# Letting the first sequence's gathers wait for fewer stores, and projecting its values one row block later instead of two

## The reference

```
y  = scale * q (gamma * state + k v^T)       # retention, 8 heads of 64, token by token
e  = argmax(x @ w_gate), or the expert of the token before where sigmoid(x @ w_local) >= 0.5
x1 = p[e] * relu(x @ w1[e]) @ w2[e]          # 8 experts, 512 -> 1024 -> 512, one for each token
for each of 4 attention experts:             # heads of 64
    ye = softmax(causal(q k^T / 8)) v wo     # q, k, v = x1 @ wq, wk, wv
    out += (top-2 gate weight of the token) * ye
```

## Time and profile before

| | |
|---|---|
| median of 3 runs | 447.73 us (447.07 to 449.4) |
| the profiled execution's own time | 449.13 us |
| its span in the trace | 447.6 us |
| mean granted TensorE clock | 0.969 |
| TensorE busy | 408.5 us (91%) |

### The profile page before, as it was taken

How to read it: one execution, slowest core, us unless ns; L and a number is a source line. 1 busy time by engine, 2 the same in 40 slices (tenths; PEclk the granted TensorE clock), 3 DMA queues, 4 the chain that set the end, 5 groups by cost and what they waited for, 6 DMA issues and landing times.

```text
span 447.6 us, 9522 instructions
## 1 busy us (share of the span) xinstructions
PE 408.5 (91%) x3224; PEld 364.9 (82%) x3225; DVE 251.7 (56%) x483; ACT 231.0 (52%) x500; POOL 78.6 (18%) x100
## 2 busy tenths in 40 slices
PE   6999894497999999999999999399899899989987
PEld 5887883396999999898989897299877789978875
DVE  1667778765474646464646465236777531676740
ACT  4766664154464646454545454134566552466643
POOL 1011113011010101000000000550188400025330
PEclk9999998589999999999999999689999999999999
DMA  8958793776867677776766840452200021220003
GB/s 266 346 187 266 260 404 138 256 233 237 281 234 252 240 265 232 252 245 253 237 232 234 287 183 23 140 166 73 70 1 1 1 95 48 70 70 0 0 0 141
DMA packets 32392, 77.47 MB, mean 173 GB/s; under 512 B 3824, under 2 KB 4080, under 8 KB 32368
## 3 DMA queue, kind: packets, MB, share of 16 engines
q1 hardware_dynamic: 25552, 57.94, 38.5%
q0 software_dynamic: 4224, 14.68, 9.6%
q10 hardware_dynamic: 2592, 4.53, 2.7%
HBM read 56.17 MB, written 17.83 MB: 165 GB/s over the span
## 4 chain that ended last, share of the span: by engine, by line
PE 77%; issue 10%; DMA 6%; POOL 2%; DVE 2%; ACT 1%; POOLq 1%; SPq 0%; ACTq 0%; DVEq 0%
PE bank L1233 7%; PE bank L1231 7%; PE bank L1232 7%; PE bank L1218 6%; PE bank L1217 6%; PE bank L1216 6%; PE bank L1335 5%; PE bank L1320 4%; PE bank L1302 3%; PE bank L1306 3%; PE bank L1277 3%; PE bank L1276 2%; PE bank L1278 2%; POOL tokens_by_expert L446 2%; DMA tokens_by_expert<-zero 2%
## 5 line engine op out<-in xcount | busy, mean ns | idle before, releaser
L1216 PE MATMUL bank<-xh,w1h 128*128 128x256 f32 x256 | 73.6, 288 | 0.9 <-DVE xl L897 0.9
L1217 PE MATMUL bank<-xl,w1h 128*128 128x256 f32 x256 | 73.4, 287 | 0.0
L1218 PE MATMUL bank<-xh,w1l 128*128 128x256 f32 x256 | 73.4, 287 | 0.0
L891 DVE TENSOR_TENSOR w2l<-raw,w2h 128x1024 fp32r<-128x1024 f32 x32 | 37.1, 1222 | 42.9 <-ACT w2h L576 42.9
L576 ACT ACTIVATE w2h<-raw 128x1024 fp32r<-128x1024 f32 x32 | 31.8, 1050 | 48.2 <-PE bank L1233 45.7
L1216 PEld LDWEIGHTS bank<-xh,w1h 128*128 128x128 f32 x256 | 50.2, 196 | 1.3 <-DVE xl L897 1.0
L1231 PE MATMUL bank<-w2h,hh 128*128 128x512 f32 x128 | 50.6, 396 | 0.0
L1217 PEld LDWEIGHTS bank<-xl,w1h 128*128 128x128 f32 x256 | 50.2, 196 | 0.3
L1218 PEld LDWEIGHTS bank<-xh,w1l 128*128 128x128 f32 x256 | 50.1, 196 | 0.0
L1233 PE MATMUL bank<-w2h,hl 128*128 128x512 f32 x128 | 49.9, 390 | 0.0
L1232 PE MATMUL bank<-w2l,hh 128*128 128x512 f32 x128 | 49.8, 389 | 0.0
(11 more groups left out here) (159 smaller groups left out, 865.6 us busy)
## 6 DMA issues: line engine op xcount, KB each, us to landing
raw<-in_w SPq DMA_DIRECT2D x64, 512.0 KB, 5.7
tokens_by_expert<-zero POOLq DMA_DIRECT2D x8, 512.0 KB, 6.2
xr<-tokens_by_expert POOLq DMA_DIRECT2D x8, 512.0 KB, 4.0
outputs_by_expert<-ysb ACTq DMA_DIRECT2D x16, 256.0 KB
kt_in<-in_kT SPq DMA_DIRECT2D x12, 256.0 KB
q_in<-in_qT SPq DMA_DIRECT2D x12, 256.0 KB
out<-osb SPq DMA_DIRECT2D x12, 256.0 KB, 2.0
v_in<-in_vR SPq DMA_DIRECT2D x11, 256.0 KB, 4.9
```

Source lines behind the costliest of these rows:

```text
L891: dve.tensor_tensor(part(low), raw[:, q, :], part(high).bitcast(F32), ALU.subtract).then_inc(w_lo, 1)
L1216: pe.matmul(to, w1h[:, dc, at], xh[:, dc, :], start=(dc == 0), stop=False)
L1217: pe.matmul(to, w1h[:, dc, at], xl[:, dc, :], start=False, stop=False)
L1218: last = pe.matmul(to, w1l[:, dc, at], xh[:, dc, :], start=False, stop=(dc == DC - 1))
```

## The change

The stores get one semaphore for each half (`ey_stored[0]`, `ey_stored[1]`), and the zeroing one of its own. While counting, VectorE keeps the counts at the end of the first sequence (`seq_count`). TensorE turns them into a row beside the final counts, VectorE copies the number of first-sequence rows in the last expert, and works out from it and from the last expert's first tile how many stores of each half GpSimd must see before the first sequence's rows are all there (`seq_i`). GpSimd loads both numbers into registers, waits for the two semaphores, and gathers the first sequence; it waits for `all_stored` only before it gathers the second. One more tile of `ys` is zeroed. ScalarE waits for the zeroing once, behind the exponentials of the routing. On TensorE and ScalarE the values of block `t` of the first sequence come after block `t + 1` is turned.

```diff
-CLEARED = MAX_TILES - E
+CLEARED = MAX_TILES - E + 1
...
+    small[:, C_HALVES:C_HALVES + TH * MAXH] = (TILE * np.arange(MAXH)[None, :] + P * np.arange(TH)[:, None]).reshape(-1)
+    small[:, C_HALVES] = -1.0
...
-            for g in range(E, MAX_TILES):
+            for g in range(MAX_TILES - CLEARED, MAX_TILES):
-                sp.dma_start(rows(ys, g * TILE, TILE)..., zero[:, :]).then_inc(ey_stored, 16)
+                sp.dma_start(rows(ys, g * TILE, TILE)..., zero[:, :]).then_inc(ys_cleared, 16)
...
             pool.wait_ge(pos2_ready, 1)
-            pool.wait_ge(all_stored, 1)
+            pool.wait_ge(seq_ready, 1)
+            tiles = [pool.value_load(seq_i[0:1, th:th + 1], min_val=E - th, max_val=MAX_TILES) for th in range(TH)]
+            for th in range(TH):
+                pool.wait_ge(ey_stored[th], 16 * tiles[th] + 16)
+            pool.sem_inc(seq_stored, 1)
+            pool.wait_ge(seq_stored, 1)
...
             gather(0)
+            pool.wait_ge(all_stored, 1)
             gather(1)
...
-                act.wait_ge(ey_stored, 16 * CLEARED + 16 * TH * (n - 1))
                 for th in range(TH):
+                    act.wait_ge(ey_stored[th], 16 * n)
...
-                    act.dma_start(rows(ys, row, P), ysb[:, th, :]).then_inc(ey_stored, 16)
+                    act.dma_start(rows(ys, row, P), ysb[:, th, :]).then_inc(ey_stored[th], 16)
...
             act.activation(exps[:, :, :], exps[:, :, :], ACT.Exp).then_inc(exps_ready, 1)
+            act.wait_ge(ys_cleared, 16 * CLEARED)
+            for th in range(TH):
+                act.sem_inc(ey_stored[th], 16)
...
-            act.wait_ge(ey_stored, 16 * CLEARED + 16 * TH * (tb + nt))
+            for th in range(TH):
+                act.wait_ge(ey_stored[th], 16 * (tb + nt) + 16)
             act.sem_inc(all_stored, 1)
...
-            for t in range(C + 2):
+            for t in range(C + 1):
                 if t < C:
                     split_x2(0, t)
-                if t >= 2:
-                    values(0, t - 2)
+                if t >= 1:
+                    values(0, t - 1)
...
+                if g == closing[C - 1]:
+                    dve.tensor_copy(seq_count[:, :], cnt[:, s, w - 1:w]).then_inc(seq_counted, 1)
...
+            dve.tensor_copy(seq_row[:, 0:1], bank[0:1, 6, 2 * E - 1:2 * E]).then_inc(seq_step, 1)
...
+            dve.wait_ge(seq_step, 1)
+            dve.tensor_tensor(seq_over[:, :], seq_row[:, 0:1].to_broadcast([1, TH * MAXH]),
+                              cst[0:1, C_HALVES:C_HALVES + TH * MAXH], ALU.is_gt).then_inc(seq_step, 1)
+            dve.wait_ge(seq_step, 2)
+            dve.reduce_sum(seq_row[:, 1:1 + TH], seq_over[:, :].rearrange("o (h k) -> o h k", h=TH), AX.X).then_inc(seq_step, 1)
+            dve.wait_ge(seq_step, 3)
+            dve.tensor_tensor(seq_i[:, :], seq_row[:, 1:1 + TH],
+                              route_f[:, R_TB + E - 1:R_TB + E].to_broadcast([1, TH]), ALU.add).then_inc(seq_ready, 1)
...
+            pe.wait_ge(seq_counted, 1)
             pe.wait_ge(cnt_ready, last_g + 1)
+            pe.matmul(bank[0:1, 6, E:2 * E], seq_count[:, :], ident[0:E, 0:E], start=True, stop=True)
...
-            for t in range(C + 2):
+            for t in range(C + 1):
                 if t < C:
                     turn_x2(0, t)
-                if t == 2:
+                if t == 1:
                     pe.wait_ge(m2_lo, 2)
-                if t >= 2:
-                    project_values(0, t - 2)
+                if t >= 1:
+                    project_values(0, t - 1)
```

More of the change, by code:

```diff
@@ L55 @@
 C_PADMIN = C_PICK + 1 + E
-C_N = C_PADMIN + E
+C_HALVES = C_PADMIN + E
+MAXH = S // TILE
+C_N = C_HALVES + TH * MAXH
 L_CAUSAL, L_KD, L_CG = 0, P, P + H
@@ L140, in build_kernel @@
         over = sb("over", [1, E * MAXT])
+        seq_count = sb("seq_count", [E, 1])
+        seq_row = sb("seq_row", [1, 1 + TH])
+        seq_over = sb("seq_over", [1, TH * MAXH])
+        seq_i = sb("seq_i", [1, TH], I32)
         ones = sb("ones", [E, GMAX * P])
@@ L241, in build_kernel @@
         ey_done, ey_ready = sem("ey_done"), sem("ey_ready")
-        ey_stored, all_stored = sem("ey_stored"), sem("all_stored")
+        ys_cleared, all_stored = sem("ys_cleared"), sem("all_stored")
+        ey_stored = [sem(f"ey_stored{th}") for th in range(TH)]
+        seq_counted, seq_step, seq_ready, seq_stored = (
+            sem("seq_counted"), sem("seq_step"), sem("seq_ready"), sem("seq_stored"))
         delta_ready, pos2_step, pos2_ready = (
@@ L397, in _ @@
             sp.wait_ge(zeroed, 1)
-            for g in range(E, MAX_TILES):
-                sp.dma_start(rows(ys, g * TILE, TILE).rearrange("(p a) n -> p (a n)", p=P), zero[:, :]).then_inc(ey_stored, 16)
+            for g in range(MAX_TILES - CLEARED, MAX_TILES):
+                sp.dma_start(rows(ys, g * TILE, TILE).rearrange("(p a) n -> p (a n)", p=P), zero[:, :]).then_inc(ys_cleared, 16)
             for s in range(XRING):
```

## The result

The changed kernel takes 444.78 us in the median of 12 runs (440.89 to 447.68), the kernel before 447.61 in 12 runs (445.3 to 449.4). The ratio is 0.9927, with a 95% interval of 0.9905 to 0.9949: 2.3 to 4.3 us faster. The longest of the 12 runs, 447.68, counts as one in the chip's slower state and isn't in the ratio. Forecast were 442.8 and a gain of 4.9. The time lies within the range of 439.8 to 445.8, but above the 441.8 to 444.5 of the forecast rival A. The gain by the ratio, 3.3 us, is two thirds of the forecast.

What follows compares the result with a forecast made beforehand. TensorE was taken as the bound, busy for 91% of the span with 77% of the chain. The profiled 449.13 - 5.0 + 0.1 gave 444.2; from the median 447.73 the same sum gave 442.8, range 439.8 to 445.8.

Steps and rivals of the forecast that it cites:

- rival A: Hand-over from experts to attention: the clock falls, gain 4 to 5.5 us, about 442.8; chance 0.50.
- The new wait opens 5.4 us earlier: GpSimd's wait before the first sequence's gathers: first gather at 277.33, TensorE's first turn at 281.20, 5.4 us earlier.
- Rival C: GpSimd's new wait opens no earlier; only the shorter lag's 0.4 us is left, 447.3; chance 0.06.
- ScalarE's copy, held by the store: ScalarE's first copy of a turned block waits for the second half's store until 282.6; first values at 284.0.
- the store gets only what the gathers leave: Late bound for the second half's store beside the gathers: its DMA part takes 2.0 us, landing at 283.2.
- half rate: Second half's store beside the gathers, with queues taking turns: slowed to about half rate at most, landing at 282.5.
- The clock: TensorE's clock at the hand-over: somewhat likelier than not to fall, then 4.3 us at half clock lose 2.15.
- Part 2: First sequence's values one block late instead of two: worth about 0.4 to 0.6 us, contained in the 284.0.
- The additions: Small added work, as zeroing, counting and register set-up, lies beside other work: +0.1 us, bounds 0 and 0.8.
- D: Early gathers hold up the second half's store on ScalarE's path; in full 1.8 us slower, 449.5, chance 0.03.
- the milder D: Gathers delay the second half's store on ScalarE's path to a landing at 285: gain 2.7, 445.0; chance 0.07.

Runs made afterwards that it cites:

- one_early: Changed kernel, but only the first block's gather goes ahead of the last stores, the second to sixth wait for all stores; ratio 0.9946 to the kernel before.
- act_free: Changed kernel, but ScalarE waits for the stores behind its second copy of a turned block instead of ahead of the first; ratio 0.9910 to the kernel before.
- fill: Changed kernel with products that nothing reads in TensorE's three gaps at the hand-over (9, 5 and 4); ratio 0.9853 to the kernel before.
- gathers_only: Changed kernel with the values two blocks late again, as before the change; ratio 0.9910 to the kernel before.
- lag_only: Kernel before with the values one block late instead of two and nothing else; ratio 1.0003 to the kernel before.
- free_fill: Changed kernel with ScalarE's wait behind its second copy and 9, 5, 0 unread products in TensorE's gaps; 438.04 us, ratio 0.9831 to the kernel before.
- adds_only: Changed kernel's additions alone: first-sequence gathers still wait for all stores and values stay two blocks late; ratio 0.9984 to the kernel before.
- fill_late: Changed kernel with unread products only behind the first turned block (5) and the second (4); ratio 0.9891 to the kernel before.
- fill_first: Changed kernel with unread products only ahead of the first turned block (9); ratio 0.9899 to the kernel before.

## Why the prediction was right in kind and too high in size

- **The new wait opens 5.4 us earlier.** Right: counted from the experts' last product, the first gather goes out 5.3 us earlier. From issue to landing 2.06 (taken: 1.98), from landing to gather 278.07 - 277.10 = 0.97 (taken: 0.90). The first turn comes 2.28 after the experts' last product; forecast 2.10. Rival C is out.
- **ScalarE's copy, held by the store, is what is late next.** Right in mechanism, and mis-sized. The landing was put at 281.86 + 0.74; with the 0.6 by which this execution was late that is 283.2, and it came at 284.2. The store took 3.7, not 2.7. The upper bound, 3.3, by "the store gets only what the gathers leave", was too low too. By "half rate", which the prediction drew from the packet turns of the Trainium skill ("DMA: Bandwidth & Descriptors", section "Queues, rings and completion order"), it would have been 2.7 by estimate; that is refuted. The turns as such are not. From 280.4 to 284.3 the profile counts 144 packets of the store in 17.5% of the 16 DMA engines' time and 179 of the gathers in 63.7%, that is 0.076 and 0.22 us a packet. If each of the store's 9 packets on an engine lets one of the gathers' pass, they need 9 x 0.30 = 2.7 us instead of 0.68, and the store 4.0: an estimate, near the 3.7. What failed is the equal share: the queue with the longer packets took the larger part, and in the five other profiles with a store beside all gathers as well (59 to 65% against 18 to 20%). No run changed the packets, so the working by turns isn't tested. The store also delayed the second gather: the turns are 1.98 apart, not 1.44. Together the first values start 5.99 after the last product instead of 4.90: 1.09 us of the missing gain. `one_early` shows that the gathers slow the store, `act_free` that the slowed store held up the first values.
- **The clock.** It fell, as in A. The size was off: 2.15 was taken for 4.3 us at 1.2 GHz, and it was 5.6; from the first values to the key projections it took 298.94 - 285.68 = 13.26 against 10.44 at full clock, 2.82. `fill` gives back 2.71, 2.53 of it behind the first values. This is 0.67 of the missing gain. 1.09 and 0.67 are the 1.76 between the forecast 5.22 (301.81 - 296.59) and the stretch's 3.46. The clock fell as well in the other three profiles with early gathers and no idle products (`gathers_only`, `one_early`, `act_free`). The two executions that can be compared, 22.69 and 22.54, show nothing of a stretch that varies by a us or two.
- **Part 2.** Forecast 0.4 to 0.6 for one block less of lag; nothing measurable. In `lag_only` the gap of 0.37 wasn't removed but came back as one of 0.41 before a later low part.
- **The additions** cost nothing that can be seen, +0.1 was taken.
- **D** happened in part: the store landed 1.7 us later than alone. It would have had to be 5.9 (287.8 against 281.86) for the gain to be gone. The median, 444.78, and the distance of the medians, 2.8, are those of the milder D (445.0 and 2.7) rather than of A. The range held because it reached beyond the milder D.
- **Comparing with a single profile.** The 449.13 and the 447.73 were used as if a stage's clock and the second tile's load were the same in each run. They aren't (the clock of 60 to 100 us: 0.79 and 0.74; the load: last section), so a part of the median's distance can't be assigned.

## What to carry to other kernels

When a wait is opened earlier, follow the in-order program of the engine that used to do the waiting: here ScalarE still stood at the old wait, one instruction ahead of the new critical work, and the transfer it stood for was slowed by the very transfers that had been let go. A gap on TensorE costs twice, by its length and by what the lower clock does to the work behind it; products that nothing reads in a gap of 2.3 us and two of about 1 gave back 2.7 us here, though the first values began only 0.2 us sooner. A small transfer beside gathers can get much less than half of the DMA engines: here 17.5% of their time against 63.7%. Where the runs of a kernel spread more than the effect, compare the length of the stretch that was changed, not the end.

## What the runs showed of the hardware that was not expected

The profiled executions differ by up to 6.4 us in when the experts end. Ten of the eleven differ only ahead of one place, TensorE's turn of the second tile: from its start to the copy of the last half 175.0 to 175.3 us pass, whatever the kernel (in `fill` 176.7). Part of it is the load of that tile, which meets the weights' loads in the routing stage. From the chain of the kernel before it took 8.89, and in other executions (chains of `lag_only`, `gathers_only`, `act_free`):

```profile
95.59 7.23 DMA xr<-tokens_by_expert
...
102.87 1.10 PE bank L1196 x8
```

```profile
94.91 7.31 DMA xr<-tokens_by_expert
...
102.27 1.09 PE bank L1231 x8
```

```profile
94.03 6.69 DMA xr<-tokens_by_expert
...
100.76 1.09 PE bank L1232 x8
```

TensorE's turn of that tile moves with it, from 103.84 before to 100.76, and so does everything behind. But the start of the load moves too, from 91.4 (`free_fill`) to 96.0 us (the changed kernel), and in `adds_only`, `fill_late` and `free_fill` the turn doesn't wait for it. How much of the spread of all runs (4 us before, 7 after) is the load's own can't be read from eleven traces.

In `fill_first` ScalarE let 1.05 us pass before its copy of the third block, which the profile puts down to nothing in the program; with one block of lag such a pause falls on TensorE. In `act_free` the same copy also starts 1.05 us behind ScalarE's instruction before it, 0.97 after its turn had ended. What causes it stays open.
